# Attention outputs and chunk-state sums on halves of the TensorE array's columns

## The reference

```python
# attention: a complex decay per channel, a 48x48 state per head
mag = np.sqrt(a_re * a_re + a_im * a_im)
scale = np.minimum(mag, 0.999) / (mag + 1e-06)
for t in range(S):
    new_re = ar * S_re - ai * S_im
    new_im = ar * S_im + ai * S_re
    S_re, S_im = new_re + k[t] (x) v[t], new_im
    y[:, :, t] = np.einsum('bhd,bhde->bhe', q[:, :, t], S_re)
# first mixer, x = y as (batch, 768, 384)
h = relu(x^T @ w_tok1) @ w_tok2;  u = x + h^T
x = u + relu(u @ w_ch1) @ w_ch2              # 384 -> 1536 -> 384
# second mixer
xn = layer_norm(x) * g_ln
out = x + relu(xn @ w_ch1') @ w_ch2'
```

## Time and profile before

| | |
|---|---|
| median of 3 runs | 970.07 us (969.06 to 970.95) |
| the profiled execution's own time | 970.12 us |
| its span, first to last instruction | 968.3 us |
| PE busy, share of the span | 886.5 us, 92% |
| mean granted TensorE clock | 0.981 of full |

### The profile page before, as it was taken

The page is one execution under the profiler, slowest core; times in us unless marked ns, Lnnn a source line. Parts: engine busy times, 40 slices in busy tenths (PEclk is TensorE's granted clock), DMA queues, the critical chain, the costliest instruction groups (busy, mean ns, idle before and its releaser), DMA issues.

```text
span 968.3 us, 13819 instructions
## 1 busy us (share of the span) xinstructions
PE 886.5 (92%) x5600; PEld 868.4 (90%) x5600; DVE 469.7 (49%) x821; ACT 414.9 (43%) x767; POOL 21.6 (2%) x39
## 2 busy tenths in 40 slices
PE   0768887899999999999999999899999999999998
PEld 0657777889999999989999999899999999999998
DVE  5866456656558557566665354425312322322121
ACT  6766356665655656646665332222211211211111
POOL 1000000000000000000000000000000000000000
PEclk9979897999999999999999999999999999999999
DMA  9826953434442544534436070000002002000000
GB/s 370 175 42 99 257 103 44 87 74 97 94 99 37 111 76 98 92 81 75 74 58 113 3 269 1 1 1 1 26 1 74 1 25 74 1 25 25 1 25 25
DMA packets 46834, 70.99 MB, mean 73 GB/s; under 512 B 5040, under 2 KB 38064, under 8 KB 46256
## 3 DMA queue, kind: packets, MB, share of 16 engines
q1 hardware_dynamic: 46768, 70.09, 31.2%
HBM read 42.86 MB, written 8.26 MB: 53 GB/s over the span
## 4 chain that ended last, share of the span: by engine, by line
PE 74%; DVE 11%; ACT 7%; DMA 4%; issue 2%; SPq 2%; DVEq 0%; ACTq 0%
PE bank L330 20%; PE bank L332 20%; PE bank L331 20%; PE bank L1229 3%; PE bank L1248 3%; DMA rows<-hats 3%; PE bank L1246 3%; PE bank L1220 2%; DMA x_u<-in_re_rows_dram 1%; PE bank L1259 1%; SPq L463 1%; ACT L594 1%; PE bank L1212 1%; DVE turned_x L1068 1%; PE bank L1314 1%
## 5 line engine op out<-in xcount | busy, mean ns | idle before, releaser
L984 DVE SCALAR_TENSOR_TENSOR hidden<-bank,hidden 128x384 fp32r<-128x384 f32 x192 | 106.9, 557 | 347.9 <-ACT hidden L693 347.8
L693 ACT ACTIVATE hidden<-bank 128x384 fp32r<-128x384 f32 x192 | 93.8, 488 | 347.8 <-PE bank L332 347.3
L330 PE MATMUL bank<-ch,hidden 128*128 128x384 f32 x576 | 198.5, 345 | 0.0
L332 PE MATMUL bank<-ch,hidden 128*128 128x384 f32 x576 | 194.1, 337 | 0.0
L331 PE MATMUL bank<-ch,hidden 128*128 128x384 f32 x576 | 193.9, 337 | 0.0
L330 PEld LDWEIGHTS bank<-ch,hidden 128*128 128x128 f32 x576 | 109.2, 190 | 0.4 <-issue 0.3
L331 PEld LDWEIGHTS bank<-ch,hidden 128*128 128x128 f32 x576 | 109.2, 190 | 0.0
L332 PEld LDWEIGHTS bank<-ch,hidden 128*128 128x128 f32 x576 | 109.0, 189 | 0.0
L330 PE MATMUL bank<-turned_x,ch 128*128 128x384 f32 x288 | 102.3, 355 | 1.9 <-DVE turned_x L1068 1.9
L332 PE MATMUL bank<-turned_x,ch 128*128 128x384 f32 x288 | 97.3, 338 | 0.0
L331 PE MATMUL bank<-turned_x,ch 128*128 128x384 f32 x288 | 97.2, 337 | 0.0
(11 more groups left out here) (165 smaller groups left out, 1555.0 us busy)
## 6 DMA issues: line engine op xcount, KB each, us to landing
rows<-hats SPq DMA_DIRECT2D x126, 128.5 KB, 4.6
a_t<-in_a_rows_dram SPq DMA_DIRECT2D x20, 384.0 KB, 4.0
qk_t<-in_qk_rows_dram SPq DMA_DIRECT2D x19, 384.0 KB, 5.6
v_t<-in_v_cols_dram SPq DMA_DIRECT2D x24, 192.0 KB, 4.1
plain_ch<-in_moe_w_ch_dram SPq DMA_DIRECT2D x6, 768.0 KB, 10.8
out_dram<-x_u SPq DMA_DIRECT2D x24, 192.0 KB, 2.0
x_kept_dram<-x_u SPq DMA_DIRECT2D x18, 192.0 KB, 3.2
x_u<-x_kept_dram SPq DMA_DIRECT2D x18, 192.0 KB, 3.2
```

The source lines that it names most:

```text
L330: nc.tensor.matmul(ps, lhs_h, rhs_h, start=first, stop=False, skip_group_check=True)
L332: return nc.tensor.matmul(ps, lhs_l, rhs_h, start=False, stop=final, skip_group_check=True)
L693: nc.scalar.activation(hid_h[:, m % NHID, :], hid_ps[m % 2][:, 0:HALF], ACT.Relu).then_inc(hidden_rounded, 1)
L984: nc.vector.scalar_tensor_tensor(out=hid_l[:, m % NHID, :], in0=hid_ps[m % 2][:, 0:HALF], scalar=0.0, in1=hid_h[:, m % NHID, :].bitcast(F3 ...
```

## The change

Where one matmul had all 128 output rows (the columns of the stationary operand), two matmuls now make 64 each: columns 0 to 63 of the stationary operand into PSUM partitions 0 to 63 and 64 to 127 into 64 to 127. In `chunk_state`, with 96, they are 64 and 32. The moving operands, the sums, their order in each output element and the semaphores stay as they were.

```diff
                 for h in range(part * HB, (part + 1) * HB):
-                    yh = y_ps[:, h * D:(h + 1) * D]
-                    last = nc.tensor.matmul(yh, masked[:, h * P:(h + 1) * P], v_head(n, h), start=True, stop=n % NT == 0)
+                    for lo in range(0, P, P // 2):
+                        last = nc.tensor.matmul(y_ps[lo:lo + P // 2, h * D:(h + 1) * D], masked[:, h * P + lo:h * P + lo + P // 2], v_head(n, h),
+                                                start=True, stop=n % NT == 0)
                     if n % NT:
-                        last = nc.tensor.matmul(yh, rows[:, n % 2, h, 0:P], state[:, n % 2, h * D:(h + 1) * D], start=False, stop=True)
+                        for lo in range(0, P, P // 2):
+                            last = nc.tensor.matmul(y_ps[lo:lo + P // 2, h * D:(h + 1) * D], rows[:, n % 2, h, lo:lo + P // 2],
+                                                    state[:, n % 2, h * D:(h + 1) * D], start=False, stop=True)
                     if busy and h % 2 == 0:
                         busy()
...
                 for h in range(H):
-                    last = nc.tensor.matmul(m_ps[0:D2, h * D:(h + 1) * D], khat[:, h * D2:(h + 1) * D2], v_head(n, h), start=True, stop=True)
+                    for lo, hi in ((0, P // 2), (P // 2, D2)):
+                        last = nc.tensor.matmul(m_ps[lo:hi, h * D:(h + 1) * D], khat[:, h * D2 + lo:h * D2 + hi], v_head(n, h), start=True, stop=True)
                 last.then_inc(chunk_states, 1)
```

## The result

The changed kernel takes 986.9 us (median of 4 runs, 986.6 to 993.0) against 970.5 before: 1.0186 times as long, 95% interval 1.0144 to 1.0227, some 16 us. Slower was right, but 43 us were forecast.

The account below looks back on a forecast made before the run. PE, busy 92% of the span, was taken to bound the kernel. Outputs +4, state sums +35, batch 0 +8 and absorbed waits -3.5 made +43.5 us on 970.1, so 1013 us, range 957 to 1037.

Parts of the forecast that it names:

- Emptying between 64 and 32 columns: State sums in slots: the array empties at each width change, 3.90 us for 1.56, +2.34 us times 15, +35 us.
- The cadence in the outputs, c = 0.048 us: Outputs in slots: time per load of 64 columns, between 0.029 and 0.058; the full and short parts sum to +4 us.
- halves fully at once: Outputs in slots: lowest of three cadences, both halves loading simultaneously, 0.029 us a load, -16 us.
- rival B: Outputs and state sums: halves independent, loads at once, no emptying between 64 and 32; 951 us, some 958 if partly absorbed; chance 0.18.
- c = 0.029: Variant of the main forecast: emptying stays, outputs give -16 for +4 and batch 0 some 3 less; 990 us.
- Batch 0, +8: Before the slots: 11.7 us from state sums and 4.6 from outputs, half of these 16.3 us exposed, +8 us.
- Absorbed in the first three slots, -3.5: First three slots: PE's 11.7 us of waits for ACT take back about half of 3 x 2.34 us, -3.5 us.
- A pass is time of the kernel in the slots: 220 to 551 us: PE busy 320.3 of 331.0 us, so a pass saved or added on PE is kernel time.
- Rival E, the clock: Stretches with waits: the gaps also lower PE's granted clock, total above 1037 us; chance 0.03.

Follow-up runs that it names:

- The reordered state sum: Changed kernel with each state sum's matmuls reordered, all 8 of 64 columns, then all 8 of 32, so one width change inside instead of 15: 968.2 us, 0.9968 of before.
- the swap on ScalarE: Kernel before the change, with ScalarE's copy of the turned k moved ahead of rounding the next tile's turns in each slot: 964.0 us, 0.9933 of before.

## Why the prediction was right in its direction and wrong in its size

- **Emptying between 64 and 32 columns, +35 us**: right. 3.95 us a state sum for 3.90; 15 times 2.39 is 36. The reordered state sum shows that it is the changes of width and nothing else. Where the Trainium skill (TensorEngine Tiling (Array Packing), Tiling Modes, Key Properties) says that a change of tiling mode drains the engine, these rows agree, for the step from 64 to 32 as well (0.12 us a change).
- **The cadence in the outputs, c = 0.048 us: the step that failed.** It measured 0.029, the low bound, "halves fully at once". Both single costs, 0.058 for a load alone and two halves at a time, stood in the prediction; I chose between the bounds by reading as "a load follows the start of the matmul ahead of it", and let a half's second pass hold up the other half. It does not: the loads of the two halves begin about 0.01 us apart, pair by pair. That put +4 where -16 belonged, 20 of the 27 us by which the forecast is off. Its own branch for c = 0.029 said 990. The Trainium skill (same page, Tiling Modes, Key Properties) says that different tiles can do their weight loads and matmuls in parallel. The prediction gave that sentence to rival B alone, for want of a row; the trace agrees with it, with 4 loads of 64 columns in 0.117 us.
- **Batch 0, +8**: +3.3 between the two traces. With c = 0.029 the prediction had about 5. As the swap on ScalarE shows, batch 0 differs by up to 8 us from trace to trace with nothing changed in it, so that this term is neither borne out nor refuted.
- **Absorbed in the first three slots, -3.5**: right, PE's waits for ScalarE there fell from 11.7 to 8.1 us. Not foreseen: 4.1 us more absorbed from 220 to 551 us.
- **A pass is time of the kernel in the slots**: true for added work beyond the 7.7 us of waits that it filled, false for most of the saved work. The prediction read 320 busy of 331 us as one bound; a second chain was a few per cent behind. That did not touch the sum, where the gain of the outputs was used up by the state sums, but it makes rival B wrong as well: its 951 would hardly have come from loads at once and no emptying, as the outputs alone on halves show (967), to which its state sums would have added 2 us of gain.
- **Rival E, the clock**: half right. The half-clock stretches behind state sums cost about 1.5 us a slot in tiles 13 to 16 of the kernel with only the state sums split, and little in the changed one.

With the measured values the sum closes: in the slots 36 - 16 - 3.6 - 4.1 = +12.3, measured +12.8 (tile 6 to tile 23). A wait of PE for VectorE (L960) grew by 1.1 us. Time at half clock shifted and changed the sum little: from 220 to 551 us there are two such stretches and none before, but in the first three slots two in place of three, so that mixer passes take 2.7 us more and scores and transposes, without their waits, about 3 us less. Why the changed kernel has so few of these and the one with whole outputs so many was not tried out.

## What to carry to other kernels

Where a product has few moving columns, 48 here, its pass is as long as its weight load, and splitting the stationary operand over equal parts of the array, part next to part in program order, halves it (0.058 us for two loads of 64 against 0.111 for one of 128). Keep one width: each change costs the emptying of the array, 0.12 to 0.13 us here, so split 96 columns into three of 32 and not into 64 and 32, and group what shares a width. And before counting a saving on an engine that is 97% busy, look for the wait that is next, here the copy of k behind an unrelated wait on ScalarE: two lines moved made the same saving worth 12.6 us in place of 4.

## What the runs showed of the hardware that I had not expected

- Loads into different halves start about 0.01 us apart and overlap fully: 4 loads of 64 columns in 0.117 us; 8 loads of 32 columns into four parts in 0.086 us. With all of one half first, 2 loads take 0.117 us, except at the seam: there passes of the upper half begin ahead of passes of the lower half that stand before them in the program (four rows of L1246, then four of L1249, from 332.19 us on).
- The emptying is also paid at a change of width from 64 to 32 in disjoint columns, and it lasts until the last matmul has all but come through: the next load begins 0.07 us before that matmul's modelled end, from 64 to 32 and back, as at L1359.
- A state sum that keeps PE busy by its busy share, but mostly in emptying, can be followed by a granted clock of 0.50 (1.2 GHz), at which a mixer pass takes 0.32 us for 0.17: 9 stretches in the slots of the kernel with whole outputs, two from 220 to 551 us in the changed one. That the emptying is the cause was not tried out.
